# The first MLP's activation formed in the PSUM bank, its linear mix given up, and the setup rearranged around it

## What is computed

```python
kv_pool = kv.reshape(B, H // r, r, W // r, r, C).mean(axis=(2, 4))
kv_flat = kv_pool.reshape(B, -1, C) @ w_sr
...
s = scale * (q @ k.transpose(0, 2, 1))
s = s - s.max(-1, keepdims=True)
a = np.exp(s)
a /= a.sum(-1, keepdims=True) + 1e-09
...
h = x @ w_in
g = np.maximum(h, 0.0) + alpha * np.minimum(h, 0.0)
...
g = h * (1.0 / (1.0 + np.exp(-1.702 * h)))
return (g @ w_out).astype(np.float32)
```

## Time and profile before

| | |
|---|---|
| median of 3 runs | 1314.45 us (1314.26 to 1314.69) |
| the profiled execution | 1313.01 us |
| its span, first to last instruction | 1311.2 us |
| granted TensorE clock, mean | 0.997 |
| busy TensorE | 1281.8 us, 98%, 5620 matmuls |
| busy VectorE | 983.3 us, 75% |
| busy ScalarE | 909.0 us, 69% |
| busy GpSimd | 413.2 us, 32% |

### The profile page before, as it was taken

How to read it: one execution, slowest core, us unless ns; L and a number is a source line. 1 busy time by engine, 2 the same in 40 slices (tenths; PEclk the granted TensorE clock), 3 DMA queues, 4 the chain that set the end, 5 groups by cost and what they waited for, 6 DMA issues and landing times.

```text
span 1311.2 us, 19249 instructions
## 1 busy us (share of the span) xinstructions
PE 1281.8 (98%) x5620; PEld 1049.3 (80%) x5620; DVE 983.3 (75%) x1743; ACT 909.0 (69%) x1576; POOL 413.2 (32%) x318
## 2 busy tenths in 40 slices
PE   4899999999999999999999999999999999999998
PEld 3667888888888888888888888888888888888886
DVE  5788868778778687687786876877868768778765
ACT  3576677776776777767767777677677777776765
POOL 2484052250440522504405225044052250440400
PEclk9899999999999999999999999999999999999999
DMA  9101000000010000000100000001000000000000
GB/s 331 56 17 33 9 24 24 16 24 24 8 32 8 24 24 16 24 24 8 32 8 24 24 16 24 24 8 32 8 24 24 16 24 24 8 24 8 17 17 8
DMA packets 17935, 36.81 MB, mean 28 GB/s; under 512 B 3456, under 2 KB 3584, under 8 KB 17280
## 3 DMA queue, kind: packets, MB, share of 16 engines
q1 hardware_dynamic: 17920, 36.62, 8.5%
HBM read 30.22 MB, written 6.39 MB: 28 GB/s over the span
## 4 chain that ended last, share of the span: by engine, by line
PE 94%; DVE 2%; ACT 2%; DMA 1%; POOL 1%; issue 0%; SPq 0%; ACTq 0%
PE ps_y L781 13%; PE ps_y L785 13%; PE ps_y L782 13%; PE ps_h L785 13%; PE ps_h L781 13%; PE ps_h L782 13%; PE ps_x L781 3%; PE ps_x L785 2%; PE ps_x L782 2%; PE ps_s L781 2%; PE ps_s L785 2%; PE ps_s L782 2%; DVE g_lo L684 1%; DVE g_hi L682 0%; DMA kv_raw<-kvT 0%
## 5 line engine op out<-in xcount | busy, mean ns | idle before, releaser
L674 DVE SCALAR_TENSOR_TENSOR g_lo<-ps_h,g_hi 128x512 fp32r<-128x512 f32 x384 | 262.4, 689 | 192.3 <-ACT g_hi L486 187.1
L373 POOL TENSOR_TENSOR s_sb<-s_sb,max_sb 128x512 f32<-128x512 f32 x138 | 178.7, 1332 | 689.3 <-DMA max_sb<-max_row 689.3
L490 ACT ACTIVATE g_full<-ps_h 128x512 f32<-128x512 f32 x384 | 229.9, 599 | 189.9 <-PE ps_h L785 179.4
L486 ACT ACTIVATE g_hi<-ps_h 128x512 fp32r<-128x512 f32 x384 | 226.2, 596 | 146.4 <-PE ps_h L785 145.7
L785 PE MATMUL ps_y<-g_lo,down_hi 128*128 128x512 f32 x768 | 299.8, 390 | 1.3 <-DVE g_lo L684 0.7
L684 DVE TENSOR_TENSOR g_lo<-g_full,g_hi 128x512 fp32r<-128x512 f32 x384 | 267.0, 701 | 44.1 <-ACT g_hi L494 37.4
L781 PE MATMUL ps_y<-g_hi,down_hi 128*128 128x512 f32 x768 | 299.3, 390 | 0.6 <-DVE g_hi L682 0.5
L782 PE MATMUL ps_y<-g_hi,down_lo 128*128 128x512 f32 x768 | 298.8, 389 | 0.0
L785 PEld LDWEIGHTS ps_y<-g_lo,down_hi 128*128 128x128 f32 x768 | 144.1, 188 | 34.5 <-DVE g_lo L684 2.8
L781 PEld LDWEIGHTS ps_y<-g_hi,down_hi 128*128 128x128 f32 x768 | 144.1, 188 | 31.6 <-issue 1.2
L385 POOL TENSOR_TENSOR exp_sum<-exp_sum,s_sb 128x512 f32<-128x512 f32 x92 | 140.6, 1528 | 89.5 <-ACT s_sb L473 88.9
(11 more groups left out here) (147 smaller groups left out, 1707.8 us busy)
## 6 DMA issues: line engine op xcount, KB each, us to landing
kv_raw<-kvT SPq DMA_DIRECT2D x12, 512.0 KB, 5.7
inv_sb<-inv_row SPq DMA_DIRECT2D x24, 256.0 KB, 3.0
outT<-out_sb SPq DMA_DIRECT2D x24, 256.0 KB, 2.0
q_raw<-qT SPq DMA_DIRECT2D x23, 256.0 KB, 2.7
max_sb<-max_row SPq DMA_DIRECT2D x23, 256.0 KB, 3.1
w_raw<-w_in SPq DMA_DIRECT2D x1, 1024.0 KB, 8.0
...
```

The costliest lines, as they stand in the source:

```text
L373: nc.gpsimd.tensor_tensor(s_sb[:, c, :], s_sb[:, c, :], max_sb[:], ALU.subtract).then_inc(diff_done, 1)
L486: nc.scalar.activation(g_hi[:, f % RING, :], ps_h[:, f % RING, :], ACT.Relu).then_inc(act_done, 1)
L490: nc.scalar.activation(g_full[:, f % RING, :], ps_h[:, f % RING, :], ACT.Gelu_apprx_sigmoid).then_inc(act_done, 1)
L674: nc.vector.scalar_tensor_tensor(g_lo[:, f % RING, :], ps_h[:, f % RING, :], 0.0, f32(g_hi[:, f % RING, :]), ALU.max, ALU.subtract).then_i ...
```

## The change

The mix goes, with all that made it (`w_in1T`, the scaled copies of `w_out`, the three matmuls a tile). In its place the activation is formed whole: h + (1 - alpha) relu(-h). For each chunk ScalarE writes relu(-h) to `m_sb` (a ring of 2), VectorE adds (1 - alpha) times that to h in the PSUM bank itself (`prelu`), and then the bank is split: `g_hi` by ScalarE, or by VectorE for the chunks in `HI_ON_DVE`, and `g_lo` by VectorE. On both engines the second step of chunk f - 1 stands behind the first step of chunk f.

GpSimd takes over the exponentials' rests (`weights_lo`), between the subtractions and the additions; `a_hi` and `a_lo` hold all six chunks now, and `EXP_AT` is three chunks earlier. In the setup, tile 0's scores, their differences and exponentials stay in six PSUM banks; `first_scores(c)` directly follows `keys_values(c)`; the maximum is spread by matmuls with a broadcast operand and copied to SBUF by ScalarE; the small loads are issued by ScalarE; the sums' matmuls of tile 0 stand partly behind its attends; GpSimd makes the rests of `w_out`. Tile 0 has its own places for the exponentials and attends.

```diff
-    EXP_AT = {7: 0, 9: 1, 10: 2, 12: 3, 13: 4, 15: 5}
-    LO_AT = {8: 0, 10: 1, 11: 2, 13: 3, 14: 4}
+    EXP_AT = {4: 0, 6: 1, 7: 2, 9: 3, 10: 4, 12: 5}
     ATTEND_AT = {11: 0, 13: 1, 14: 2}
+    HI_ON_DVE = (3, 6, 8, 11)
...
+    FIRST_EXP_AT = {8: 0, 9: 1, 11: 2, 12: 3, 13: 4, 15: 5}
+    FIRST_ATTEND_AT = {14: 0, 15: 1}
...
+        banks0 = (ps_h[:, 3, :], ps_h[:, 0, :], ps_h[:, 1, :], ps_h[:, 2, :], ps_s[:], ps_y1[:])
...
+            def weights_lo(b, c):
+
+                pool.wait_ge(a_hi_made, b * KC + (KC + c + 1))
+                nc.gpsimd.tensor_tensor(a_lo[:, c, :], s_sb[:, c, :], f32(a_hi[:, c, :]), ALU.subtract).then_inc(a_split, 1)
...
             for i in range(PIECES):
-                scale_rows(w_raw[1], alpha_sb, down_full, i).then_inc(w_scaled, 1)
+                first_up_lo(i)
             for i in range(PIECES):
-                pool.wait_ge(w_scaled, i + 1)
-                scale_rows(w_raw[1], one_less, w_raw[1], i).then_inc(w_scaled, 1)
-            first_up_lo(2)
-            first_up_lo(3)
+                first_down_lo(i)
+            for i in range(PIECES):
+                second_lo(i)
             subtract_max(0)
-            second_lo(0)
+            for c in range(KC):
+                weights_lo(0, c)
             queries_lo(2)
-            second_lo(1)
-            sum_exponentials(0)
+            second_lo(4)
+            add_exponential(0, 1)
+            add_exponential(0, 2)
+            second_lo(5)
...
+            def tile(t, score):
+                subtract_max(t)
+                weights_lo(t, 0)
+                weights_lo(t, 1)
+                weights_lo(t, 2)
+                add_exponential(t, 1)
+                weights_lo(t, 3)
+                add_exponential(t, 2)
+                weights_lo(t, 4)
+                weights_lo(t, 5)
+                if score:
+                    queries_lo(t + 2)
+                add_exponential(t, 3)
+                add_exponential(t, 4)
+                add_exponential(t, 5)
...
-            def relu_hi(t, f):
+            def below_zero(t, f):
                 act.wait_ge(up_done, t * UPS + (f + 1))
-                nc.scalar.activation(g_hi[:, f % RING, :], ps_h[:, f % RING, :], ACT.Relu).then_inc(act_done, 1)
+                if f >= M_RING:
+                    act.wait_ge(full_done, t * CH + (f - M_RING + 1))
+                nc.scalar.activation(m_sb[:, f % M_RING, :], ps_h[:, f % RING, :], ACT.Relu, scale=-1.0).then_inc(m_made, 1)
+
+            def prelu_hi(t, f):
+                if f not in HI_ON_DVE:
+                    act.wait_ge(full_done, t * CH + (f + 1))
+                    nc.scalar.copy(g_hi[:, f % RING, :], ps_h[:, f % RING, :]).then_inc(hi_made, 1)
...
                 for f in range(LAG, CH):
-                    relu_hi(t, f)
-                    if attend and f in EXP_AT:
-                        exponentials(t + 1, EXP_AT[f], t)
-                        exponentials_hi(t + 1, EXP_AT[f])
+                    below_zero(t, f)
+                    prelu_hi(t, f - 1)
+                    if attend and f in exp_at:
+                        exponentials(t, exp_at[f])
+                        exponentials_hi(t, exp_at[f])
...
+            for i in range(PIECES):
+                first_up_hi(i)
+            max_to_sbuf()
             for c in range(KC + 1):
                 if c < KC:
-                    exponentials(0, c)
+                    first_exponentials(c)
                 if c >= 1:
-                    exponentials_hi(0, c - 1)
+                    first_exponentials_hi(c - 1)
+                if c == 2:
+                    first_down_hi(0)
+                if c == 4:
+                    first_down_hi(1)
...
-            def relu_lo(t, f):
-                dve.wait_ge(act_done, t * UPS + (f + 1))
-                nc.vector.scalar_tensor_tensor(g_lo[:, f % RING, :], ps_h[:, f % RING, :], 0.0,
-                                               f32(g_hi[:, f % RING, :]), ALU.max, ALU.subtract).then_inc(g_split, 1)
+            def prelu(t, f):
+                dve.wait_ge(m_made, t * CH + (f + 1))
+                nc.vector.scalar_tensor_tensor(ps_h[:, f % RING, :], m_sb[:, f % M_RING, :], one_less[:, f:f + 1],
+                                               ps_h[:, f % RING, :], ALU.mult, ALU.add).then_inc(full_done, 1)
+
+            def prelu_parts(t, f):
+                if f in HI_ON_DVE:
+                    dve.wait_ge(full_done, t * CH + (f + 1))
+                    nc.vector.tensor_copy(g_hi[:, f % RING, :], ps_h[:, f % RING, :]).then_inc(dve_hi_made, 1)
+                    dve.wait_ge(dve_hi_made, t * len(HI_ON_DVE) + (his_before(f, True) + 1))
+                else:
+                    dve.wait_ge(hi_made, t * HIS_ACT + (his_before(f, False) + 1))
+                nc.vector.tensor_tensor(g_lo[:, f % RING, :], ps_h[:, f % RING, :], f32(g_hi[:, f % RING, :]),
+                                        ALU.subtract).then_inc(g_split, 1)
...
                 for f in range(LAG, CH):
-                    relu_lo(t, f)
+                    prelu(t, f)
+                    prelu_parts(t, f - 1)
+                    if first(t) and f == FIRST_SUMS_AT:
+                        first_inverse()
                     if score and f == QUERIES_AT:
                         queries_hi(t + 1)
...
-                    if attend and f in LO_AT:
-                        weights_lo(t + 1, LO_AT[f])
-                for c in range(len(LO_AT), KC if attend else 0):
-                    weights_lo(t + 1, c)
-
+                prelu_parts(t, CH - 1)
                 divide(t)
...
-            first_max_at = {7: 1, 9: 2}
+            first_max_at = {7: 1, 9: 2, 11: 3}
...
+                if c == 9:
+                    chunk_max(0, 1)
...
-                passes(ps_y1[:], mix_hi[:], mix_lo[:], x_hi[:], x_lo[:], False, False)
                 for f in range(CH - LAG, CH):
                     down(t, 0, f)
...
             for c in range(KC):
-                if c >= 1:
-                    first_scores(c - 1)
                 keys_values(c)
+                first_scores(c)
                 if c >= 1:
                     scores(0, c - 1)
-            first_scores(KC - 1)
-            scores(0, KC - 1)
...
+            for c in range(4):
+                first_attend(c)
+            first_sums(0)
+            first_attend(4)
+            first_sums(1)
+            first_attend(5)
+            for c in range(2, 5):
+                first_sums(c)
+            first_sums(5).then_inc(sums0_made, 1)
+            scores(0, KC - 1)
             for f in range(LAG):
                 up(0, 0, f)
-            pe.wait_ge(mix_split, 1)
+
+            pe.wait_ge(sum_steps, 1)
```

More of the change, by code:

```diff
@@ L31, in attention_mlp_kernel @@
     w_in1: bass.AP,
-    w_in1T: bass.AP,
     w_out1: bass.AP,
@@ L224, in attention_mlp_kernel @@
         y_split = sem("y_split")
-        w_in = [sem(f"w_in{i}") for i in range(5)]
+        w_in = [sem(f"w_in{i}") for i in range(4)]
         kv_in = [sem(f"kv_in{i}") for i in range(KV_RING)]
@@ L264, in casts_before, with his_before @@
             return sum((j in CAST_ON_ACT) == on_act for j in range(f))
+        HIS_ACT = CH - len(HI_ON_DVE)
+        def his_before(f, on_dve):
+            return sum((j in HI_ON_DVE) == on_dve for j in range(f))
         block = ctx.enter_context(nc.Block())
@@ new lines, in keys_values_hi, with begin_max, max_to_sbuf @@
+                if not last:
+                    act.wait_ge(kv_out, 2 * c + 1)
+                    nc.scalar.copy(k_hi[:, cols(c)], k_full[:, c % 2, :]).then_inc(k_hi_made, 1)
+                act.wait_ge(kv_out, 2 * c + (1 if last else 2))
+                nc.scalar.copy(v_hi[:, c, :], v_full[:, c % 2, :]).then_inc(v_hi_made, 1)
+            def begin_max():
+                act.wait_ge(scores0_done, 1)
+                nc.scalar.copy(running_max0[:], banks0[0]).then_inc(max0_begun, 1)
+            def max_to_sbuf():
+                act.wait_ge(max0_spread, 1)
+                nc.scalar.copy(max_row0[:], ps_y2[:]).then_inc(max_row0_made, 1)
@@ L464, in scores_to_sbuf @@
                 nc.scalar.copy(s_sb[:, c, :], next_score_bank(b, c)).then_inc(scores_out, 1)
-            def exponentials(u, c, before=0):
-                if first(u):
-                    act.wait_ge(diff0_done, c + 1)
-                    if c >= len(exp0_banks):
-                        act.wait_ge(a_split, c - len(exp0_banks) + 1)
-                else:
-                    act.wait_ge(diff_done, before * KC + (c + 1))
-                nc.scalar.activation(exponential_of(u, c), scores_of(u, c), ACT.Exp).then_inc(exp_done, 1)
@@ new lines, in first_exponentials_hi, with exponentials, exponentials_hi @@
+            def first_exponentials_hi(c):
+                act.wait_ge(exp_done, c + 1)
+                nc.scalar.copy(a_hi[:, c, :], banks0[c]).then_inc(a_hi_made, 1)
+            def exponentials(b, c):
+                act.wait_ge(diff_done, b * KC + (c + 1))
```

(27 more changed lines are left out.)

350 lines of the change are left out of this document (158 added, 192 removed).

## The result

The changed kernel takes 1362.18 us (median of 4 runs, 1361.13 to 1363.32), the kernel before 1314.36 beside it (1313.25 to 1314.69). The ratio is 1.0364, 95% interval 1.0352 to 1.0377: slower by 47.8 us. The prediction had the sign right, and was far too small: +19, and 1362 lies outside its range.

The account below looks back on a forecast made before the run. TensorE was taken as the bound (231 matmuls a tile at 0.227 us). 1313.0 + 19.4 (22 tiles, 0.88 longer) - 0.6 (setup, tile 0, tile 23) = 1331.8; the median, 1.4 higher, gives 1333 us, range 1298 to 1344.

Parts of the forecast that it names:

- a lead of one microsecond too few: First MLP, chunks 3 to 12: VectorE needs 14.4 us, ScalarE 14.0, TensorE gives 12.3; the lead lends about 1 us.
- TensorE stays the bound: Rival: VectorE operations between `prelu(3)` and lo 8 cost less, the stall shrinks or goes, TensorE still bounds; 1298 us, chance 0.27.
- short casts: Rival: VectorE's casts from PSUM take 0.43 us, stall 1.0 or 0.63; 1320 to 1313 us; chance 0.13 shared with the addition's lock.
- the addition holds the divide: Rival: GpSimd's last addition holds `y_hi` and `y_lo`, up to 0.55 us a tile; 1310 or 1304; chance 0.13 shared with short casts.
- Sum: 0.12 + 0.78 + 0.27 + 0.39 = 1.56 us of stall in a tile: TensorE's waits for hi or lo of chunks 3, 6 and 8; against 0.68 saved, a tile 0.88 us longer.
- the walk: Step-by-step timing of ScalarE and VectorE from chunk 3 of the first MLP, giving 1.56 us of TensorE stall a tile.
- After chunk 10 the attends at 11, 13 and 14 (0.68 us each) let all catch up: End of the first MLP: three attends' matmuls give the other engines time, so no stall was counted after chunk 10.
- if nothing else moves: Condition on the saving from removing three mix matmuls a tile: 0.68 us a tile, 16.3 us in all.
- dearer `prelu`: Rival: `prelu` reads and writes one bank, 0.10 us more on each of seven, stall 2.3; 1349 us, chance 0.10.
- -0.6: Sum for setup (-1.3, first `up` at 51.0), tile 0 (saves 0.68, pays some 1.6, GpSimd +0.5) and tile 23 (-0.7).

Follow-up runs that it names:

- Experiment 9: The changed kernel with the third attend after `up(15)` instead of behind chunk 14: 1356.69 us, ratio 1.0311.
- experiment 1: The kernel before without its three mix matmuls a tile, leaving out the first MLP's linear part: 1300.78 us, ratio 0.9892.
- Experiment 6: The kernel before with `weights_lo` on GpSimd (last rest later), earlier exponentials, and an added in-bank VectorE step per chunk, rests one chunk behind: 1326.03 us, ratio 1.0085.
- experiment 5: The changed kernel with `prelu` empty and ScalarE writing relu(h) into the bank, so without the activation's negative side: 1318.52 us, ratio 1.0032.
- experiment 4: The changed kernel with all sixteen hi casts of the first MLP on ScalarE, none on VectorE: 1361.75 us, ratio 1.0365.

## Why the prediction was right in sign and short in size

**Right.** The bound before, and the mechanism. TensorE's 231 matmuls at 0.227; a lead of one microsecond too few between chunks 3 and 12; the two engines holding each other around exponential 1; stalls at chunks 3, 6 and 8, in just these places. The cast from PSUM: 0.68 taken, 0.68 to 0.69 measured, so neither 0.43 nor its rivals. The Trainium skill's one element a cycle ("VectorE: DVE Perf Modes", Why PSUM operands drop a tier), 0.66 by the page's formula, is close. The lo subtraction: 0.69 and 0.60 from start to start. GpSimd's last addition does not reach the divide. The rivals "TensorE stays the bound", "short casts" and "the addition holds the divide" all fall.

**Wrong in size: the sum of the stall.** The step is "Sum: 0.12 + 0.78 + 0.27 + 0.39 = 1.56 us of stall in a tile". By the starts of one tile it is 0.37 at chunk 3, 0.96 at chunk 6 (predicted 1.05 in two parts), 0.48 at chunk 8, and 0.59 at the end: 2.40, and 54.30 - 51.86 gives 2.44. So the three places that the walk named hold 1.81 instead of 1.56, and a fourth one holds 0.59 instead of nothing. Two terms are missing in the sum.

- "After chunk 10 the attends at 11, 13 and 14 (0.68 us each) let all catch up": they do until chunk 13, but `down(14)` and `down(15)` have nothing behind `up(15)` to lend them time. 0.59 us a tile, 13 us in all. The mix's matmuls had stood there. The prediction counted them as 0.68 saved "if nothing else moves", and took no note that their place was the lead of the last three chunks. Experiment 9 puts an attend there and takes the stall away.
- The uncovered weight load. I had `down(f)` wait until its operand was there and then go on at 0.227. In the trace a late `g_hi` or `g_lo` costs 0.11 more each, also when the wait itself is nearly nothing. At chunk 3 that is most of the 0.37. No run here changes this alone: it is read from the rows of loads and starts.

`prelu` was sized at 0.69 and 0.60. It takes 0.75, and the next starts 0.65 later. The rival "dearer `prelu`" had 0.10 more and 1349; measured are 0.05 to 0.06 more. In the tight chunks 6 and 8, where that would show, the stalls are 0.96 and 0.48, together the 1.44 that the walk had (0.78, 0.27, 0.39): there errors cancel. `prelu` and the loads add, and `q_hi`, which the walk gave 0.90 after GpSimd's subtraction, took 0.48. It was not even on the path: what held chunk 6 is ScalarE's `below_zero(7)` behind exponential 1.

**Wrong: what the matmuls are worth.** 0.68 taken, 0.58 measured (experiment 1): 2 us in all.

**Wrong: the setup and tile 0, "-0.6".** They and tile 23 measured +9.0 (6.8 and 2.2). The first `up` came at 52.57, predicted 51.0. Tile 0's first MLP was costed like the others, plus 0.5 for GpSimd. But there VectorE also has the maxima among the chunks, and `prelu` stands with them ahead of the rests: the first three of five waits of 0.68 to 1.24 us, where the kernel before had one of 0.64. At the last, 78.46, it is ScalarE that is late: casts of the second MLP's weights (two of them in chunks 10 and 11) and the exponentials stand among its steps, and VectorE waits 1.11 us for `below_zero(12)`. Experiment 6 has +6.25 by VectorE's step alone, and experiment 5 still +4.2 without it: either engine's added work is enough to spoil this stretch, and their shares can't be told apart. That the first `up` came at 52.57 and not at 51.0 is within what single executions differ by. Tile 23 was put at -0.7, for it has no exponentials; but its VectorE casts still stall, as experiment 4 shows.

So of the 29 us between forecast and result, 22 are the middle tiles (1.88 longer instead of 0.88, 22 times) and 9.6 are the setup, tile 0 and the last tile, less the 2.5 by which the profiled spans differ more than the medians.
